# A GELU layer's output product: one float32 matmul each in place of three of rounded parts

## The chip, the cores and the metric

The kernel runs on one core of a Trainium2 chip. The metric is the device time of one execution in microseconds (us); lower is better. A core has TensorE (PE, whose weight loads are listed apart as PEld), VectorE (DVE), ScalarE (ACT), GpSimd (POOL) and SyncE (SP, which issues the DMAs). Matmuls write PSUM, which has eight banks of 128 partitions x 512 float32.

## The reference

A decayed attention (4 batches, 8 heads, 768 steps, head size 48) feeds a soft mixture of experts, and that feeds the layer that the change is in:

```python
def _moe2_ref(x, w_in, w_out):            # x: 3072 x 384, w_in: 384 x 2048, w_out: 2048 x 384
    h = x @ w_in
    g = h * (1.0 / (1.0 + np.exp(-1.702 * h)))
    return (g @ w_out).astype(np.float32)
```

All inputs and the output are float32.

## The kernel before, in words

The program is written out by hand, one instruction stream for each engine, with semaphores between them: `wait_ge(s, n)` blocks the engine until semaphore `s` has reached `n`, `.then_inc(s, 1)` raises it when the instruction is done. No scheduler moves anything. There are three stages: the attention, the mixture of experts, and the layer above, which is the last. Ahead of the last stage the kernel has folded `w_in` with the experts' output into `mst` (128 x 2048) and holds the combine weights of all tokens in `cst` (128 x 3072), so that h of 128 hidden channels and 512 tokens is one matmul.

The last stage goes through 3072 tokens in 6 blocks of TB = 512, and in each block through FF = 2048 hidden channels in FC = 16 chunks of 128. A step is one chunk of one block, so there are 96 steps; T = 32 of them (two blocks) are one pass of `two_blocks`, and three passes (ITS = 3) make the stage. In step s:

- PE computes h of step s+2 into bank 6 or 7 by one matmul (`hidden`).
- ACT turns it into g by the GELU activation, into one of NG = 4 slots of `gact` (`gelu`), which lies in the tile `ring`.
- DVE splits g of step s (`split`): `g_hi` is g rounded to float32r, `g_lo` is g minus `g_hi`, rounded likewise. Both are float32r, a 32-bit type with fewer mantissa bits for TensorE.
- PE adds w_out^T g to the output, 128 output channels (CM = 3 groups `o`) by 512 tokens in each of three banks: for each group wo_hi·g_hi, wo_lo·g_hi and wo_hi·g_lo, so 9 matmuls of 128 x 128 by 128 x 512.

`w_out` lies raw in `wraw` (two slots of `ring`, loaded by four DMAs on SP's queue, one semaphore `ld_wout` for each quarter). In the first block ACT rounds one chunk of it per step to `wo_hi` (`round_wout`) and DVE subtracts it to `wo_lo` (`low_wout`). PE's banks 0 to 2 and 3 to 5 take turns by block. After a block ACT copies the three banks to `ostage` (`evacuate`) and SP stores them. At the very end the last step runs group by group, so that ACT and DVE can copy each finished bank (`last_done`).

float32r matmuls also stand in `hidden` and in the two products with `spread`. All the other matmuls of the kernel, apart from the bfloat16 ones of `stay_warm`, take plain float32 operands; `t.transpose` is a matmul with the identity.

Of the kernel before, what the change touches and what calls it, by code (L numbers as in the profile page):

```python
# [16 lines left out]
def decay_attention_soft_moe_gelu_kernel(nc, rk_in, w0_in, nat_in, u_in, phi_in, w1_in, w2_in, win_in, wout_in, out_t):  # L17
# [17 lines left out]
    CM = phi_in.shape[1]  # L35
    DM = CM * P
# [6 lines left out]
    FC = FF // P  # L43
    NT = B * NC
    N = NT * P
    TB = 512
    T = 2 * FC
    ITS = N // (2 * TB)
# [7 lines left out]
    with top:  # L56
        def sb(stack, name, shape, dt=F32):
            return stack.enter_context(nc.sbuf_tensor(name, shape, dt))

        def sem(name):  # L60
            return top.enter_context(nc.semaphore(name))
# [73 lines left out]


        gen3 = ExitStack()
        wo_hi = sb(gen3, "wo_hi", [P, FC, DM], F32R)
        wo_lo = sb(gen3, "wo_lo", [P, FC, DM], F32R)
        NG = 4  # L140
        gact = ring[:, 1, 0:NG * TB].rearrange("p (a t) -> p a t", a=NG)
        g_split = sb(gen3, "g_split", [P, NG, 2, TB], F32R)
        g_hi, g_lo = (g_split[:, :, q, :] for q in range(2))
        ostage = ring[:, 0, 0:2 * CM * TB].rearrange("p (a o t) -> p a o t", a=2, o=CM)
        gen3.close()
        gen2.close()
# [1 line left out]
        wraw = ring[:, 6:8, :].rearrange("p a m -> p (a m)")  # L148

        bank = [top.enter_context(nc.psum_tensor(f"bank{i}", [P, BANK], F32)) for i in range(8)]  # L150
# [49 lines left out]
        FQ = FC // WQ  # L200
        ld_win = [sem(f"ld_win{m}") for m in range(CM)]
        ld_wout = [sem(f"ld_wout{q}") for q in range(WQ)]
# [47 lines left out]
        spread_set = sem("spread_set")  # L250
        spread_done = sem("spread_done")
        m_out = [sem(f"m_out{i}") for i in range(2)]
        wohi_done = sem("wohi_done")
        wolo_done = sem("wolo_done")

        h_done = sem("h_done")
        g_done = sem("g_done")
        ghi_done = sem("ghi_done")
        glo_done = sem("glo_done")
        step_done = sem("step_done")  # L260
        o_out = [sem(f"o_out{i}") for i in range(2)]
        last_done = sem("last_done")
# [195 lines left out]
        def _(act):  # L458
            a = nc.scalar
# [143 lines left out]
                combine_out(q, act, lambda dst, src: a.activation(dst, src, ACT.Copy), ct_act)  # L603

            a.preload_act_table(ACT.Gelu_apprx_sigmoid)
            def round_wout(f):
                if f % FQ == 0:
                    act.wait_ge(ld_wout[f // FQ], 16)
                a.activation(wo_hi[:, f, :], wraw[:, DM * f:DM * (f + 1)], ACT.Copy).then_inc(wohi_done, 1)

            act.wait_ge(l2_done, 1)
            combine(0)
            combine(1)
            act.wait_ge(m_done, 1)
            a.activation(mhi[:, :], bank[0][:, :], ACT.Copy).then_inc(m_hi, 1)
            combine(2)
            round_wout(0)
            for q in range(0, WQ, 2):
                act.wait_ge(spread_done, q + 1)
                a.activation(mst[:, q * BANK:(q + 1) * BANK], bank[SPREAD[q]][:, :], ACT.Copy).then_inc(m_out[0], 1)  # L620

            def gelu(it, s):
                act.wait_ge(h_done, T * it + s + 1)
                act.wait_ge(glo_done, T * it + s + 1)
                a.activation(gact[:, s % NG, :], bank[6 + s % 2][:, :], ACT.Gelu_apprx_sigmoid).then_inc(g_done, 1)  # L625

            def evacuate(it, par):
                act.wait_ge(step_done, T * it + FC * (par + 1) + NG)
                act.wait_ge(stored[par], 16 * it + 16)
                for o in range(CM):  # L630
                    a.activation(ostage[:, par, o, :], bank[3 * par + o][:, :], ACT.Copy).then_inc(o_out[par], 1)

            def two_blocks(it, last=False, rounding=False):
                for s in range(T):
                    if s + 2 < T or not last:
                        gelu(it, s + 2)
                    if rounding and s + 2 < FC:
                        round_wout(s + 2)
                    if rounding and s < 2:
                        combine(4 + s)  # L640
                    if s == FC:
                        evacuate(it, 0)
                if not last:
                    evacuate(it, 1)

            gelu(0, 0)
            gelu(0, 1)
            round_wout(1)
            two_blocks(0, rounding=True)
            with act.Fori(1, ITS - 1) as it:  # L650
                two_blocks(it)
            two_blocks(ITS - 1, last=True)
# [6 lines left out]
        @block.vector  # L659
        def _(dve):  # L660
            v = nc.vector
            dve.sem_inc(glo_done, NG)
            dve.sem_inc(logit_out, 1)
            v.memset(lw[:, :, D:HOFF], 0.0).then_inc(const_dve, 1)
            for q in (5, 6, 7):
# [178 lines left out]
            v.tensor_copy(si4[:, :], bank[6][:, 0:DM]).then_inc(so_out, 1)  # L844
            dve.wait_ge(so_t, 1)
            v.tensor_copy(soT[:, :, :], bank[7][:, 0:CM * NS].rearrange("p (m s) -> p m s", m=CM)).then_inc(so_ready, 1)
            def low_wout(f):
                dve.wait_ge(wohi_done, f + 1)
                v.tensor_tensor(wo_lo[:, f, :], wraw[:, DM * f:DM * (f + 1)], wo_hi[:, f, :].bitcast(F32),
                                ALU.subtract).then_inc(wolo_done, 1)  # L850

            dve.wait_ge(m_hi, 1)
            v.tensor_tensor(mlo[:, :], bank[0][:, :], mhi[:, :].bitcast(F32), ALU.subtract).then_inc(m_lo, 1)
            combine_out(3, dve, v.tensor_copy, ct_dve)
            low_wout(0)
            for q in range(1, WQ, 2):
                dve.wait_ge(spread_done, q + 1)
                v.tensor_copy(mst[:, q * BANK:(q + 1) * BANK], bank[SPREAD[q]][:, :]).then_inc(m_out[1], 1)

            def split(it, s):  # L860
                dve.wait_ge(g_done, T * it + s + 3)
                dve.wait_ge(step_done, T * it + s + 1)
                v.tensor_copy(g_hi[:, s % NG, :], gact[:, s % NG, :]).then_inc(ghi_done, 1)  # L863
                dve.wait_ge(ghi_done, T * it + s + 1)
                v.tensor_tensor(g_lo[:, s % NG, :], gact[:, s % NG, :], g_hi[:, s % NG, :].bitcast(F32), ALU.subtract).then_inc(glo_done, 1)  # L865

            for s in range(T):
                split(0, s)
                if s + 1 < FC:
                    low_wout(s + 1)  # L870
            with dve.Fori(1, ITS) as it:
                for s in range(T):
                    split(it, s)

            dve.wait_ge(last_done, 2)
            dve.wait_ge(stored[1], 16 * ITS)
# [2 lines left out]
        @block.tensor  # L879
        def _(pe):  # L880
            t = nc.tensor
            pe.sem_inc(step_done, NG)
            pe.sem_inc(lgt_done, 1)
            pe.sem_inc(logit_done, 1)

# [176 lines left out]
            last = Step(B - 1, PPB - 2)  # L1062
# [18 lines left out]
            for n in range(OLD):  # L1081
# [5 lines left out]
                if n == 3 * G4:  # L1087
                    pe.wait_ge(new_exp, 1)
                    for j in range(2):
                        ins = t.transpose(bank[2][:, G3 * NS * j:G3 * NS * (j + 1)], e_new[0:G3 * NS, P * j:P * (j + 1)],  # L1090
                                          ident[0:G3 * NS, 0:G3 * NS])
# [3 lines left out]
                ins = dispatch(bank[6], n, n < G4, n >= OLD - G4)  # L1095
            ins.then_inc(old_slots, 1)
            pe.wait_ge(new_weights, 1)
            for n in range(OLD, NT):
                ins = dispatch(bank[7], n, n < OLD + G4, n >= NT - G4)
# [6 lines left out]
            for m in range(CM):  # L1106
                ins = t.matmul(bank[0][:, NS * m:NS * (m + 1)], si4[:, P * m:P * (m + 1)], sel[:, 0:NS], start=True, stop=True)
# [94 lines left out]
            def two_blocks(it, last=False):  # L1202
                for s in range(T):
                    par, f = divmod(s, FC)
                    if s + 2 < T or not last:
                        hidden(it, s + 2)
                    if s == 0:
                        for i in range(2):
                            pe.wait_ge(m_out[i], WQ // 2)
                        pe.wait_ge(ct_dve, 1)  # L1210
                    if s == 4:
                        pe.wait_ge(ct_act, 5)
                    if f == 0:
                        pe.wait_ge(o_out[par], CM * it + 1)
                    pe.wait_ge(ghi_done, T * it + s + 1)
                    if last and s == T - 1:
                        pe.wait_ge(glo_done, T * it + s + 1 + NG)
                        for o in range(CM):
                            for wo, g in ((wo_hi, g_hi), (wo_lo, g_hi), (wo_hi, g_lo)):
                                ins = t.matmul(bank[3 * par + o][:, :], wo[:, f, P * o:P * (o + 1)], g[:, s % NG, :],  # L1220
                                               start=False, stop=(g is g_lo))
                            ins.then_inc(last_done, 1)
                        continue
                    for wo in (wo_hi, wo_lo):
                        if s < FC:
                            pe.wait_ge(wohi_done if wo is wo_hi else wolo_done, s + 1)
                        for o in range(CM):
                            t.matmul(bank[3 * par + o][:, :], wo[:, f, P * o:P * (o + 1)], g_hi[:, s % NG, :],  # L1228
                                     start=(f == 0 and wo is wo_hi), stop=False)
                    pe.wait_ge(glo_done, T * it + s + 1 + NG)  # L1230
                    for o in range(CM):
                        ins = t.matmul(bank[3 * par + o][:, :], wo_hi[:, f, P * o:P * (o + 1)], g_lo[:, s % NG, :],  # L1232
                                       start=False, stop=(f == FC - 1))
                    ins.then_inc(step_done, 1)

            hidden(0, 0)
            hidden(0, 1)
# [48 lines left out]
```

## Time and profile before

| | before |
|---|---|
| runs (us) | 406.31, 401.21, 403.70 |
| median of 3 | 403.7 |
| the profiled execution's own time | 402.38 |
| its span, first to last instruction | 400.7 |
| PE busy in the span | 392.0 us, 98% |
| mean granted TensorE clock | 1.000 |

The profiled execution's time is its span and 1.7 us around it. Times in the profile count from the start of the span. PE being busy 98% is modelled from overlapping matmuls: the mean ns of a matmul is its latency from start to end, and a new one starts before the last has ended, so the pace is read from starts, or from the length of a run of matmuls.

### The profile page before, as it was taken

What the parts mean: (1) busy time and instruction counts of PE and PEld (TensorE: products, weight loads), DVE (VectorE), ACT (ScalarE), POOL (GpSimd) and SP (SyncE); (2) the same over time, 40 slices, a digit from 0 to 9 for tenths busy, and PEclk for the clock granted to TensorE, in tenths of its full rate; (3) what the DMA queues carried; (4) which work ended last, traced back from release to release, by engine and by line L of the source; (5) the groups of instructions that cost most, each with busy time, mean ns of one, the idle gap of its engine ahead of it and who ended that gap; (6) DMA issues with size and microseconds to landing.
All of it is one profiled execution on the core that took longest, in us unless ns stands there. A gap on an engine that the chain in (4) does not pass through costs nothing.

```text
span 400.7 us, 8754 instructions
## 1 busy us (share of the span) xinstructions
PE 392.0 (98%) x3306; PEld 313.1 (78%) x3306; DVE 242.5 (61%) x453; ACT 188.7 (47%) x418; POOL 49.1 (12%) x50
## 2 busy tenths in 40 slices
PE   7998999999999999999999999999999999999996
PEld 6877888888888743458888888888888888888885
DVE  5877886977978766148675445454454545445451
ACT  5777877787788523055444222422332242223221
POOL 3522442224322200000000000000000000000000
PEclk9999999999999999999999999999999999999999
DMA  7999999899999899950000200200020020002002
GB/s 293 413 360 393 334 371 344 298 398 353 327 358 346 345 408 400 416 213 2 1 2 2 77 2 0 79 0 1 0 79 0 0 79 2 0 2 79 0 2 79
DMA packets 15859, 68.66 MB, mean 171 GB/s; under 512 B 1744, under 2 KB 2896, under 8 KB 14800
## 3 DMA queue, kind: packets, MB, share of 16 engines
q1 hardware_dynamic: 15824, 68.18, 44.5%
q8 instruction: 24, 0.39, 0.4%
q14 instruction: 11, 0.09, 0.1%
HBM read 63.46 MB, written 4.72 MB: 170 GB/s over the span
## 4 chain that ended last, share of the span: by engine, by line
PE 86%; DMA 7%; DVE 3%; issue 1%; ACT 1%; SPq 1%; DVEq 0%; ACTq 0%
PE bank L1228 32%; PE bank L1232 16%; PE bank L1199 6%; DMA rk<-rk_in 5%; PE bank L1008 4%; PE bank L894 4%; PE bank L1035 4%; PE bank L1128 3%; PE bank L1148 3%; PE bank L1027 2%; DMA nat<-nat_in 2%; PE bank L990 2%; PE bank L974 2%; PE bank L953 2%; PE bank L914 2%
## 5 line engine op out<-in xcount | busy, mean ns | idle before, releaser
L625 ACT ACTIVATE ring<-bank 128x512 f32<-128x512 f32 x96 | 57.4, 598 | 138.4 <-PE bank L1199 138.3
L863 DVE CAST g_split<-ring 128x512 fp32r<-128x512 f32 x96 | 40.8, 425 | 88.4 <-ACT ring L625 88.4
L1228 PE MATMUL bank<-g_split,wo_hi 128*128 128x512 f32 x285 | 80.1, 389 | 0.0
L1228 PE MATMUL bank<-g_split,wo_lo 128*128 128x512 f32 x285 | 80.0, 389 | 0.0
L1232 PE MATMUL bank<-g_split,wo_hi 128*128 128x512 f32 x285 | 80.0, 389 | 0.0
L865 DVE TENSOR_TENSOR g_split<-ring,g_split 128x512 fp32r<-128x512 f32 x96 | 66.5, 693 | 3.3
L1228 PEld LDWEIGHTS bank<-g_split,wo_hi 128*128 128x128 f32 x285 | 53.4, 188 | 11.2 <-DVE g_split L863 0.2
L1232 PEld LDWEIGHTS bank<-g_split,wo_hi 128*128 128x128 f32 x285 | 53.5, 188 | 11.1
L1228 PEld LDWEIGHTS bank<-g_split,wo_lo 128*128 128x128 f32 x285 | 53.5, 188 | 11.1
L1199 PE MATMUL bank<-cst,mst 128*128 (+1 forms) x96 | 37.4, 391 | 0.0
L443 POOL TENSOR_TENSOR nat<-nat 128x576 f32<-128x576 f32 x16 | 22.6, 1414 | 78.9 <-DVE nat L735 45.9
L715 DVE TENSOR_TENSOR at<-bank,causal 128x512 f32<-128x512 f32 x48 | 30.0, 680 | 1.5 <-PE bank L1008 1.5
L520 ACT ACTIVATE sc<-tsum,fdec 112x48 f32<-112x48 f32 x80 | 23.6, 372 | 9.9 <-DVE tsum L709 9.9
L1008 PE MATMUL bank<-rk 48*128 48x128 f32 x384 | 25.7, 280 | 0.0
L894 PE MATMUL bank<-tri,lw 128*112 128x129 f32 x192 | 25.2, 280 | 0.3 <-ACT lw L470 0.3
L1035 PE MATMUL bank<-at,nat 128*48 128x128 f32 x384 | 24.3, 276 | 0.0
L894 PEld LDWEIGHTS bank<-tri,lw 128*112 128x112 f32 x192 | 21.9, 177 | 2.4 <-ACT lw L470 0.6
L1008 PEld LDWEIGHTS bank<-rk 48*128 48x128 f32 x384 | 22.7, 187 | 1.2 <-issue 0.4
L698 DVE TENSOR_TENSOR rk<-rk,pinv 112x768 f32<-112x768 f32 x15 | 14.5, 966 | 14.7 <-DMA rk<-rk_in 9.8
L447 POOL TENSOR_TENSOR nat<-nat,ub 128x576 f32<-128x576 f32 x16 | 22.6, 1411 | 3.1 <-DVE tsum L709 2.0
L1035 PEld LDWEIGHTS bank<-at,nat 128*48 128x48 f32 x384 | 20.2, 123 | 3.0 <-issue 3.0
L1199 PEld LDWEIGHTS bank<-cst,mst 128*128 128x128 f32 x96 | 17.9, 188 | 3.9 <-ACT mst L620 0.3
(162 smaller groups left out, 429.7 us busy)
## 6 DMA issues: line engine op xcount, KB each, us to landing
nat<-nat_in SPq DMA_DIRECT2D x32, 576.0 KB, 5.8
rk<-rk_in SPq DMA_DIRECT2D x16, 768.0 KB, 7.5
ring<-w_in SPq DMA_DIRECT2D x16, 768.0 KB, 7.4
w2a<-w_in SPq DMA_DIRECT2D x4, 1536.0 KB, 8.9
out_t<-ring SPq DMA_DIRECT2D x5, 768.0 KB, 3.5
ring<-w_in SPq DMA_DIRECT2D x6, 512.0 KB, 7.2
ring<-win_in SPq DMA_DIRECT2D x3, 1024.0 KB, 7.9
ring<-wout_in SPq DMA_DIRECT2D x4, 768.0 KB, 13.6
```

The costliest lines, as they stand in the source:

```text
L443: g.tensor_tensor(rb, rb, kb, ALU.mult).then_inc(bonus_done, 1)
L520: ins = a.activation(sc[0:DP, c, :], tsum[0:DP, :].rearrange("p (e c) -> p e c", e=D)[:, :, c], ACT.Copy, scale=fdec[0:DP, c:c + 1])
L625: a.activation(gact[:, s % NG, :], bank[6 + s % 2][:, :], ACT.Gelu_apprx_sigmoid).then_inc(g_done, 1)
L715: v.tensor_tensor(at[:, 4 * q:4 * q + 4, :], bank[2 + q][:, :].rearrange("p (u t) -> p u t", u=4), causal[:, :].unsqueeze(1).to_broadcast( ...
L863: v.tensor_copy(g_hi[:, s % NG, :], gact[:, s % NG, :]).then_inc(ghi_done, 1)
L865: v.tensor_tensor(g_lo[:, s % NG, :], gact[:, s % NG, :], g_hi[:, s % NG, :].bitcast(F32), ALU.subtract).then_inc(glo_done, 1)
L894: return t.matmul(bank[c // G3][0:DP, (c % G3) * (P + 1):(c % G3 + 1) * (P + 1)], lw[:, c, 0:DP], tri[:, :], start=True, stop=True)
L1008: ins = t.matmul(bank[2 + u // 4][:, P * (u % 4):P * (u % 4 + 1)], k[rows, P * c:P * (c + 1)], r[rows, P * c:P * (c + 1)], start=True, sto ...
L1035: ins = t.matmul(bank[6 + q][half:half + D, P * (c // 2):P * (c // 2 + 1)], nat[s.slot][:, 0, HD * c + D * h:HD * c + D * (h + 1)], at[:, ...
L1199: t.matmul(bank[6 + s % 2][:, :], mst[:, P * f:P * (f + 1)], cst[:, bass.ds((2 * it + n) * TB, TB)], start=True, stop=True).then_inc(h_don ...
L1228: t.matmul(bank[3 * par + o][:, :], wo[:, f, P * o:P * (o + 1)], g_hi[:, s % NG, :], start=(f == 0 and wo is wo_hi), stop=False)
L1232: ins = t.matmul(bank[3 * par + o][:, :], wo_hi[:, f, P * o:P * (o + 1)], g_lo[:, s % NG, :], start=False, stop=(f == FC - 1))
```

## The change

It drops the tiles `wo_hi`, `wo_lo` and `g_split` and everything that fills them (`round_wout` on ACT, `low_wout` and `split` on DVE). PE multiplies `wraw` with `gact` directly, both plain float32, with one matmul for each group `o`. PE now waits for `gelu` itself (`g_done`) and, in the first block, for the quarter of w_out (`ld_wout`).

```diff
-            def split(it, s):
-                dve.wait_ge(g_done, T * it + s + 3)
-                dve.wait_ge(step_done, T * it + s + 1)
-                v.tensor_copy(g_hi[:, s % NG, :], gact[:, s % NG, :]).then_inc(ghi_done, 1)
-                dve.wait_ge(ghi_done, T * it + s + 1)
-                v.tensor_tensor(g_lo[:, s % NG, :], gact[:, s % NG, :], g_hi[:, s % NG, :].bitcast(F32), ALU.subtract).then_inc(glo_done, 1)
...
             def gelu(it, s):
                 act.wait_ge(h_done, T * it + s + 1)
-                act.wait_ge(glo_done, T * it + s + 1)
...
-                    pe.wait_ge(ghi_done, T * it + s + 1)
...
-                    for wo in (wo_hi, wo_lo):
-                        if s < FC:
-                            pe.wait_ge(wohi_done if wo is wo_hi else wolo_done, s + 1)
-                        for o in range(CM):
-                            t.matmul(bank[3 * par + o][:, :], wo[:, f, P * o:P * (o + 1)], g_hi[:, s % NG, :],
-                                     start=(f == 0 and wo is wo_hi), stop=False)
-                    pe.wait_ge(glo_done, T * it + s + 1 + NG)
-                    for o in range(CM):
-                        ins = t.matmul(bank[3 * par + o][:, :], wo_hi[:, f, P * o:P * (o + 1)], g_lo[:, s % NG, :],
-                                       start=False, stop=(f == FC - 1))
-                    ins.then_inc(step_done, 1)
+                    if s < FC and f % FQ == 0:
+                        pe.wait_ge(ld_wout[f // FQ], 16)
+                    pe.wait_ge(g_done, T * it + s + 3)
+                    for o in range(CM):
+                        ins = t.matmul(bank[3 * par + o][:, :], wraw[:, DM * f + P * o:DM * f + P * (o + 1)], gact[:, s % NG, :],
+                                       start=(f == 0), stop=(f == FC - 1))
+                        if last and s == T - 1:
                             ins.then_inc(last_done, 1)
+                    if not (last and s == T - 1):
+                        ins.then_inc(step_done, 1)
```

On PE, one step of the last stage stood like this before; `cst,mst` is `hidden`, the three rows of three are the products of rounded parts, and the ISA and REGISTER_ALU rows set up waits.

```order
L1199 MATMUL bank<-cst,mst 128x512
L1214 ISA
L1215 REGISTER_ALU
L1228 MATMUL bank<-g_split,wo_hi 128x512 x3
L1228 MATMUL bank<-g_split,wo_lo 128x512 x3
L1230 REGISTER_ALU
L1232 MATMUL bank<-g_split,wo_hi 128x512 x3
```

The same step in the changed program, to the next `hidden`; both operands of the product now lie in `ring`, and a row counts matmuls as they are written in the program:

```order
L1158 MATMUL bank<-cst,mst 128x512
L1173 ISA
L1178 MATMUL bank<-ring 128x512 x3
L1156 REGISTER_ALU
L1158 MATMUL bank<-cst,mst 128x512
```

The nine matmuls after `hidden` have become three. On DVE, the end of the folding and the first step of the last stage stood like this before:

```order
L853 TENSOR_TENSOR mlo<-bank,mhi 128x512
L307 CAST cst<-bank 128x512
L849 TENSOR_TENSOR wo_lo<-ring,wo_hi 128x384
L858 CAST mst<-bank 128x512 x2
L863 CAST g_split<-ring 128x512
L865 TENSOR_TENSOR g_split<-ring,g_split 128x512
```

And in the changed program, to the end of DVE's stream:

```order
L829 TENSOR_TENSOR mlo<-bank,mhi 128x512
L299 CAST cst<-bank 128x512
L833 CAST mst<-bank 128x512 x2
L837 COPY ring<-bank 128x512
L56 UNCONDITIONAL_BRANCH
```

The subtraction for `wo_lo` that stood ahead of the two copies to `mst` is gone, and after these copies DVE has only the last bank's copy left.

## Rows read from the trace of the kernel before

**Rows 1.** The page: busy time and instructions of each engine; granted clock in 40 slices

```profile
PE 392.0 (98%) x3306; PEld 313.1 (78%) x3306; DVE 242.5 (61%) x453; ACT 188.7 (47%) x418; POOL 49.1 (12%) x50
...
PEclk9999999999999999999999999999999999999999
```

**Rows 2.** The page: shares of the span in the chain that ended last

```profile
PE 86%; DMA 7%; DVE 3%; issue 1%; ACT 1%; SPq 1%; DVEq 0%; ACTq 0%
```

**Rows 3.** Stage table (x: instructions; then clock, DMA share, GB/s): last stage, its 80 steady steps

```profile
180.20:397.40 217.20, 217.17 (x958) 179.58 (x957) 114.19 (x207) 71.15 (x127) 0.00 (x0) 1.00 0.05 19
182.33:362.40 180.07, 180.07 (x796) 149.16 (x795) 95.76 (x175) 59.58 (x107) 0.00 (x0) 1.00 0.05 18
```

**Rows 4.** Timeline of PE: an early step, the next `hidden`, and one 80 steps on

```profile
182.33 0.39 PE L1199 MATMUL bank<-cst,mst 128*128 x1
182.56 0.84 PE L1228 MATMUL bank<-g_split,wo_hi 128*128 128x512 f32 x3
183.24 0.84 PE L1228 MATMUL bank<-g_split,wo_lo 128*128 128x512 f32 x3
183.92 0.84 PE L1232 MATMUL bank<-g_split,wo_hi 128*128 128x512 f32 x3
184.60 0.39 PE L1199 MATMUL bank<-cst,mst 128*128 x1
...
363.67 0.39 PE L1199 MATMUL bank<-cst,mst 128*128 128x512 f32 x1
```

**Rows 5.** Matmul groups by shape (stationary partitions*columns, moving): count, busy, latency

```profile
L1228 PE MATMUL bank<-g_split,wo_hi 128*128 128x512 f32 x285 | 80.1, 389 | 0.0
L1128 PE MATMUL bank<-ring,slotT 128*32 128x512 f32 x96 | 10.7, 594 | 0.1
L1174 PE MATMUL bank<-ring,soT 128*32 128x512 f32 x24 | 2.8, 596 | 0.0
L1148 PE MATMUL bank<-w2a,hidT 128*32 128x384 f32 x64 | 5.8, 489 | 0.0
L894 PE MATMUL bank<-tri,lw 128*112 128x129 f32 x192 | 25.2, 280 | 0.3 <-ACT lw L470 0.3
L1156 PE MATMUL bank<-ident,cs 128*128 128x128 f32 x24 | 3.6, 281 | 0.0
```

**Rows 6.** Timeline of PE: uninterrupted runs of float32 matmuls, start and length

```profile
147.59 7.07 PE L1128 MATMUL bank<-ring,slotT 128*32 128x512 f32 x64
...
159.07 2.76 PE L1148 MATMUL bank<-w2a,hidT 128*32 128x384 f32 x32
...
172.91 2.78 PE L1174 MATMUL bank<-ring,soT 128*32 128x512 f32 x24
...
67.08 1.57 PE L894 MATMUL bank<-tri,lw 128*112 128x129 f32 x12
```

**Rows 7.** Weight loads by tile: duration ns min/median/max, first and last start, forms

```profile
L894 PEld LDWEIGHTS bank<-tri,lw x192: 172/177/177, 4.4 to 124.8; 128*112 128x112 f32 x192
L1008 PEld LDWEIGHTS bank<-rk x384: 182/188/188, 9.2 to 132.6; 48*128 48x128 f32 x192
L1228 PEld LDWEIGHTS bank<-g_split,wo_hi x285: 186/188/189, 180.2 to 393.4; 128*128 128x128 f32 x143
L891 PEld LDWEIGHTS bank<-ones x33: 95/99/181, 1.3 to 178.1; 128*128 128x128 bf16 x33
```

**Rows 8.** Groups of DVE and ACT in the last stage; idle before, and its releaser

```profile
L865 DVE TENSOR_TENSOR g_split<-ring,g_split 128x512 fp32r<-128x512 f32 x96 | 66.5, 693 | 3.3
L863 DVE CAST g_split<-ring 128x512 fp32r<-128x512 f32 x96 | 40.8, 425 | 88.4 <-ACT ring L625 88.4
L849 DVE TENSOR_TENSOR wo_lo<-ring,wo_hi 128x384 fp32r<-128x384 f32 x16 | 8.9, 557 | 7.7 <-ACT wo_hi L609 7.7
L625 ACT ACTIVATE ring<-bank 128x512 f32<-128x512 f32 x96 | 57.4, 598 | 138.4 <-PE bank L1199 138.3
L609 ACT ACTIVATE wo_hi<-ring 128x384 fp32r<-128x384 f32 x16 | 8.3, 519 | 0.0
L631 ACT ACTIVATE ring<-bank 128x512 f32<-128x512 f32 x15 | 7.9, 601 | 2.9 <-PE bank L1232 2.9
```

**Rows 9.** The chain in order of time into the last stage: start, us, what

```profile
178.48 0.73 PE bank L1199 x2
179.21 0.87 PE bank L1156 x8
180.08 0.24 PE bank L1199
180.32 1.49 PE bank L1228 x6
```

**Rows 10.** Issues and landings of the four DMAs that load w_out

```profile
L388 SPq DMA_DIRECT2D ring<-wout_in x4: 422/432/543, 160.2 to 161.7; - x4
...
DMA to landing us min/median/max: 11.5/13.6/15.6
```

More of the change, by code:

```diff
@@ L137, in decay_attention_soft_moe_gelu_kernel @@
         gen3 = ExitStack()
-        wo_hi = sb(gen3, "wo_hi", [P, FC, DM], F32R)
-        wo_lo = sb(gen3, "wo_lo", [P, FC, DM], F32R)
         NG = 4
         gact = ring[:, 1, 0:NG * TB].rearrange("p (a t) -> p a t", a=NG)
-        g_split = sb(gen3, "g_split", [P, NG, 2, TB], F32R)
-        g_hi, g_lo = (g_split[:, :, q, :] for q in range(2))
         ostage = ring[:, 0, 0:2 * CM * TB].rearrange("p (a o t) -> p a o t", a=2, o=CM)
@@ L252, in decay_attention_soft_moe_gelu_kernel @@
         m_out = [sem(f"m_out{i}") for i in range(2)]
-        wohi_done = sem("wohi_done")
-        wolo_done = sem("wolo_done")
         h_done = sem("h_done")
         g_done = sem("g_done")
-        ghi_done = sem("ghi_done")
-        glo_done = sem("glo_done")
         step_done = sem("step_done")
@@ L605, in _ @@
             a.preload_act_table(ACT.Gelu_apprx_sigmoid)
[L606 to L609, printed above, removed]
             act.wait_ge(l2_done, 1)
@@ L616, in _ @@
             combine(2)
-            round_wout(0)
             for q in range(0, WQ, 2):
@@ L623, in gelu @@
                 act.wait_ge(h_done, T * it + s + 1)
-                act.wait_ge(glo_done, T * it + s + 1)
                 a.activation(gact[:, s % NG, :], bank[6 + s % 2][:, :], ACT.Gelu_apprx_sigmoid).then_inc(g_done, 1)
             def evacuate(it, par):
-                act.wait_ge(step_done, T * it + FC * (par + 1) + NG)
+                act.wait_ge(step_done, T * it + FC * (par + 1))
                 act.wait_ge(stored[par], 16 * it + 16)
@@ L631, in evacuate, with two_blocks @@
                     a.activation(ostage[:, par, o, :], bank[3 * par + o][:, :], ACT.Copy).then_inc(o_out[par], 1)
-            def two_blocks(it, last=False, rounding=False):
+            def two_blocks(it, first=False, last=False):
                 for s in range(T):
@@ L636, in two_blocks @@
                         gelu(it, s + 2)
-                    if rounding and s + 2 < FC:
-                        round_wout(s + 2)
-                    if rounding and s < 2:
+                    if first and s < 2:
                         combine(4 + s)
@@ L647, in _ @@
             gelu(0, 1)
-            round_wout(1)
-            two_blocks(0, rounding=True)
+            two_blocks(0, first=True)
             with act.Fori(1, ITS - 1) as it:
@@ L661, in _ @@
             v = nc.vector
-            dve.sem_inc(glo_done, NG)
             dve.sem_inc(logit_out, 1)
@@ L846, in _ @@
             v.tensor_copy(soT[:, :, :], bank[7][:, 0:CM * NS].rearrange("p (m s) -> p m s", m=CM)).then_inc(so_ready, 1)
[L847 to L850, printed above, removed]
             dve.wait_ge(m_hi, 1)
@@ L854, in _ @@
             combine_out(3, dve, v.tensor_copy, ct_dve)
-            low_wout(0)
             for q in range(1, WQ, 2):
@@ L858, in _ @@
                 v.tensor_copy(mst[:, q * BANK:(q + 1) * BANK], bank[SPREAD[q]][:, :]).then_inc(m_out[1], 1)
-            def split(it, s):
-                dve.wait_ge(g_done, T * it + s + 3)
-                dve.wait_ge(step_done, T * it + s + 1)
-                v.tensor_copy(g_hi[:, s % NG, :], gact[:, s % NG, :]).then_inc(ghi_done, 1)
-                dve.wait_ge(ghi_done, T * it + s + 1)
-                v.tensor_tensor(g_lo[:, s % NG, :], gact[:, s % NG, :], g_hi[:, s % NG, :].bitcast(F32), ALU.subtract).then_inc(glo_done, 1)
[L867 to L873, printed above, removed]
             dve.wait_ge(last_done, 2)
@@ L881, in _ @@
             t = nc.tensor
-            pe.sem_inc(step_done, NG)
             pe.sem_inc(lgt_done, 1)
@@ L1214, in two_blocks @@
                         pe.wait_ge(o_out[par], CM * it + 1)
-                    pe.wait_ge(ghi_done, T * it + s + 1)
-                    if last and s == T - 1:
-                        pe.wait_ge(glo_done, T * it + s + 1 + NG)
-                        for o in range(CM):
-                            for wo, g in ((wo_hi, g_hi), (wo_lo, g_hi), (wo_hi, g_lo)):
-                                ins = t.matmul(bank[3 * par + o][:, :], wo[:, f, P * o:P * (o + 1)], g[:, s % NG, :],
-                                               start=False, stop=(g is g_lo))
-                            ins.then_inc(last_done, 1)
-                        continue
-                    for wo in (wo_hi, wo_lo):
-                        if s < FC:
-                            pe.wait_ge(wohi_done if wo is wo_hi else wolo_done, s + 1)
-                        for o in range(CM):
-                            t.matmul(bank[3 * par + o][:, :], wo[:, f, P * o:P * (o + 1)], g_hi[:, s % NG, :],
-                                     start=(f == 0 and wo is wo_hi), stop=False)
-                    pe.wait_ge(glo_done, T * it + s + 1 + NG)
-                    for o in range(CM):
-                        ins = t.matmul(bank[3 * par + o][:, :], wo_hi[:, f, P * o:P * (o + 1)], g_lo[:, s % NG, :],
-                                       start=False, stop=(f == FC - 1))
-                    ins.then_inc(step_done, 1)
+                    if s < FC and f % FQ == 0:
[5 more added lines that the diff above has]
+                        if last and s == T - 1:
+                            ins.then_inc(last_done, 1)
+                    if not (last and s == T - 1):
+                        ins.then_inc(step_done, 1)
             hidden(0, 0)
```

## The prediction

> **What bounds the kernel now.** I read the page first: PE is busy 98% of the span at the full granted clock [rows 1], and the chain that ended last lies 86% on PE [rows 2]. That share alone doesn't say what the last stage is worth, so I went on to the stage table: from 180.20 to 397.40, PE is busy 217.17 of 217.20 us, at clock 1.00, with DVE at 114 us and ACT at 71 us [rows 3]. More than half of the execution is this stage, and in it nothing but PE's own pace counts. The pace is read from the starts, since the listed 389 ns is a latency [rows 5]: `hidden` starts at 182.33 and, 80 steps later, at 363.67 [rows 4]. That is 2.267 us for a step of ten float32r matmuls, **0.2267 us for each**, and one early step is as long (184.60 − 182.33 = 2.27). The reader is to see that no step waits for the split, for rounding or for a store, so work taken from DVE and ACT gives nothing back.
>
> **What the change removes from DVE and ACT.** 96 pairs of cast and subtraction (40.8 + 66.5 us), 16 subtractions (8.9 us) and 16 roundings on ACT (8.3 us) go [rows 8]. All of it lies beside a PE that is never idle, so its worth on the path is 0. ACT keeps 96 GELUs of 0.598 us [rows 8] and waits 138 us in all for `hidden`; it stays far from being late. PE's new wait is for `gelu` of step s, but `hidden(s+2)`, which stands ahead of it in PE's queue, already waited for the same count. Nothing new is queued behind it, and this costs 0. PE's wait for a quarter of w_out costs 0 as well: the last of the four loads is issued at 161.7 and the longest takes 15.6 us to land [rows 10], so all are there by 177.3, before the first product near 180.3 [rows 9].
>
> **What it does to PE.** 96 × 9 float32r matmuls go and 96 × 3 float32 ones come; `hidden` (96, float32r) stays. The question is the price of a float32 product of 128 x 128 by 512. No row has that shape with the array's full width, so I take it apart.
>
> First, how many instructions one product is. The program has 6 matmuls at L894 for each of 16 pairs, 96 in all, and the trace lists 192; at L1174 it has 12 and the trace lists 24; at L1128, 48 and 96 [rows 5]. float32 products run as two instructions. float32r products don't: 285 of a possible 288 at L1228 are listed for wo_hi [rows 5], and the stage has 958 instructions on PE for ten a step [rows 3]. Transposes don't either (24 written, 24 listed at L1156), but they aren't products.
>
> Second, the pace of one such instruction. At L1128 four matmuls of 32 output columns run side by side, so 64 instructions are 16 turns of the moving 512 columns: (7.07 − 0.594) / 15 = 0.4317 us a turn. At L1174, 6 turns of the same: (2.78 − 0.596) / 5 = 0.4368. With 384 columns at L1148, 8 turns: (2.76 − 0.489) / 7 = 0.3244 [rows 5, 6]. From 384 to 512 columns the cost grows by 0.00084 us a column, about twice what a float32r column can cost (0.2267 / 512 = 0.00044). For the full width the nearest row is L894 with 112 output columns and 129 moving: (1.57 − 0.280) / 11 = 0.1173 [rows 5, 6], where the line through L1128 and L1148 gives 0.3244 − 255 × 0.00084 = 0.1107 (an estimate). The wide weights thus add some 0.0066. So the ends for a turn at full width are 0.432 (nothing added) and 0.443 (L1174 with 0.0066 added), and I take **0.437**, L1128 with most of that added.
>
> The sum for a step: 3 products × 2 × 0.437 = 2.622 against 9 × 0.2267 = 2.040, that is +0.582 us; for 96 steps **+55.9 us**. By the ends of the turn it is 96 × (2.592 − 2.040) = +53.0 and 96 × (2.658 − 2.040) = +59.3.
>
> The Trainium skill (TensorE: Matmul & The Clock Gate, Back-to-back issue gap) gives the start-to-start of a warm matmul as N / 2.4 + 2.5 ns. For N = 512 that is 216 ns, 11 ns less than this trace's 227 for float32r. An estimate by that page for a product of four passes is 4 × 213.3 + 2 × 2.5 = 858 ns, for which the sum would be 96 × (3 × 0.858 − 2.040) = +51 us instead of +56. The measured pace decides, and so the sum goes by the rows above.
>
> **Both ends of the stage.** At the opening DVE's 0.557 us subtraction ahead of the copies to `mst` goes, and so does the first cast. But the chain shows PE working without a gap through the transposes and `hidden` into the first product [rows 9], so at most some 0.4 us comes back, and I take 0. At the end the last product's latency is 594 instead of 389 ns [rows 5], +0.2 us. Copies and store follow as before. ACT's three copies after a block and a GELU take 3 × 0.601 + 0.598 = 2.4 us [rows 8], longer than a step of 2.27 and shorter than one of 2.85; there was no gap on PE before, and there will be none.
>
> The sum against the profiled execution's own 402.38 us: 402.38 + 55.9 + 0.2 = **458.5 us**. The median of the runs shown is 403.7, so the profiled one is 0.3% quicker than that; the runs lie between 401.2 and 406.3.
>
> **Rivals.**
>
> *A product costs less than three float32r matmuls (faster).* The mechanism is that a wide float32 product runs as one instruction of 0.437, as the transposes do (24 of 24 at L1156). A step is then 3 × 0.437 + 0.227 = 1.54 us, 70 us less in all: 332 us. Should the operands be taken as float32r after all, so that the change doesn't do what it says, it is 4 × 0.2267 = 0.907 a step, 131 us less: 272 us. The case turns to faster from the point at which a product costs under 3 × 0.2267 = 0.680, so 0.340 an instruction if there are two. For it speaks only that no row has the full shape. Against it: every float32 line that isn't a transpose is listed twice, L894 with 112 columns among them, and all turns of 512 take 0.432 or more [rows 5, 6]. Chance 4%.
>
> *Weight loads come into the open (slower still).* A float32 product loads two sets of weights. A load takes 0.188 us [rows 7] and is hidden now, since a float32r matmul and its load together take 0.2267. If the second half's load couldn't run under the first half's matmul, 288 × 0.188 = 54 us come on top: 512 us; if none could, 108 us: 566 us. Against it: at L894 a float32 instruction comes every 0.117 us although its load alone takes 0.177, and a longer matmul gives more cover, not less. Chance 4%. The Trainium skill (the same page, Part 3, The mechanism) states that a weight load overlaps a running matmul only if it is for another row group, which would be this rival in full, and would hold for float32r too; the trace speaks against it. It also says (Weight-path perf modes) that the fast weight load is on when the type isn't FP32. The bfloat16 load takes 99 ns here and float32r's 188, as float32's [rows 7], so the change loses no fast load.
>
> *The clock falls to its lower level, 1.2 GHz.* It was at 2.4 GHz (1.00) in every slice [rows 1, 3], in float32 stages as in float32r ones, with PE always at work. If the whole stage ran at half clock, 96 × 2.85 = 273 us would be added: about 731 us. Chance 1%.
>
> **How the numbers follow.** The forecast has 90%: 458.5 us, slower. The ends of the turn and of the opening give 402.38 + 53.0 − 0.4 = 455 and 402.38 + 59.3 + 0.2 = 462; the runs of before reach 0.3% below the profiled one and 1.0% above, which makes 453.6 to 466.5. The skill's price lies a little under that, and I let the range go from 451 to 467. The faster rival has 4%, exposed loads 4%, the clock 1%, and 1% is for something that cancels most of it. That makes faster by over 2% 0.04, within 2% (about what a measurement can tell from no change here) 0.01, slower 0.95.
>
> **What the profile after would show.** The product's line has twice its 288 matmuls, near 576, with a latency near 594 ns. `hidden` starts every 2.85 us. PE stays without idle time until the end, the stage is about 273 us long, DVE is idle in it but for one copy, and ACT's wait for `hidden` grows by some 55 us. Everything ahead of 180 us stays as it is. I am wrong if that line has 288 entries, if steps are under 2.27 us, if PE idles between products for ACT or for its own weight loads, or if the granted clock leaves 1.00.

## The result, and the profile after

| | before | changed |
|---|---|---|
| median (us) | 403.32 (4 runs, 401.21 to 406.31) | 454.31 (4 runs, 454.09 to 455.22) |
| the profiled execution | 402.38, span 400.7 | 455.22, span 453.5 |

The ratio is **1.126** (95% interval 1.119 to 1.134): the change makes the kernel 51 us slower. The forecast was 458.5 us in a range of 451 to 467.

The first lines are the changed kernel's page: busy time and instructions of each engine, the granted clock in 40 slices, the chain's shares, and the groups of the product and of the GELU.

```profile
PE 444.9 (98%) x3018; PEld 261.0 (58%) x3018; DVE 127.9 (28%) x245; ACT 182.4 (40%) x402; POOL 49.0 (11%) x50
...
PEclk9999999999999999999999999999999999999999
...
PE 89%; DMA 6%; DVE 3%; issue 1%; SPq 1%; ACT 1%; DVEq 0%; POOL 0%; POOLq 0%
PE bank L1178 55%; DMA rk<-rk_in 6%; PE bank L1158 5%; PE bank L967 4%; PE bank L853 4%; PE bank L994 3%; PE bank L1087 2%; PE bank L1107 2%; PE bank L986 2%; PE bank L933 2%; PE bank L949 2%; PE bank L912 1%; PE bank L892 1%; PE bank L873 1%; PE bank L850 1%; PE bank L1019 1%
...
L1178 PE MATMUL bank<-ring 128*128 128x512 f32 x576 | 262.5, 592 | 0.0
...
L610 ACT ACTIVATE ring<-bank 128x512 f32<-128x512 f32 x96 | 57.2, 597 | 193.6 <-PE bank L1158 193.5
```

Against [rows 1]: DVE's busy time has halved, 98% of the span is still PE, and the new line alone holds 55% of the chain. The 288 products are 576 instructions. ACT waits 193.5 us for `hidden` where it waited 138.3 [rows 8]: what was taken from the other engines has become their idle time.

The next lines are the changed kernel's timeline of PE: two steps, and the end, where 18 instructions of the product run without a `hidden` between them.

```profile
183.56 0.80 PE L1158 MATMUL bank<-cst,mst 128*128 x1
184.20 2.74 PE L1178 MATMUL bank<-ring 128*128 128x512 f32 x6
186.37 0.79 PE L1158 MATMUL bank<-cst,mst 128*128 x1
...
441.78 0.79 PE L1158 MATMUL bank<-cst,mst 128*128 128x512 f32 x1
442.41 7.89 PE L1178 MATMUL bank<-ring 128*128 128x512 f32 x18
```

From 183.56 to 441.78 are 92 steps: **2.807 us a step** against 2.267 in [rows 4]. That is +0.540, and 96 × 0.540 = +51.8 us, the whole of the loss. The last line gives the pace of one instruction undisturbed: (7.89 − 0.592) / 17 = **0.4293 us**, so 0.859 us a product where three float32r matmuls took 0.680. What is left for `hidden` is 2.807 − 6 × 0.4293 = 0.231, a little over its 0.2267 among its own kind.

The weight loads of the changed kernel, in the timeline with what each load engine waited for, don't come into the open:

```profile
300.14 0.19 PEld L1178 LDWEIGHTS bank<-ring 128*128 128x128 f32 x1 [0.24 <-issue]
300.57 0.19 PEld L1178 LDWEIGHTS bank<-ring 128*128 128x128 f32 x1 [0.24 <-issue]
```

Each lasts 0.19 us and starts 0.43 us after the last, with 0.24 us of idle time between, while the matmuls show no gap (0.0 us idle at L1178 in the page above): there is one load for each of a product's two instructions, and it runs under the instruction before it.

### The profile page after: what moved, and what is told of

Same layout as the page of the kernel before. It is cut to its first block, busy times and chain, and to the rows that moved or that the text cites. A ratio compares the mean times of both kernels' runs of the same rounds, so it can differ in the third digit from the quotient of the medians.

```text
span 453.5 us, 7646 instructions
## 1 busy us (share of the span) xinstructions
PE 444.9 (98%) x3018; PEld 261.0 (58%) x3018; DVE 127.9 (28%) x245; ACT 182.4 (40%) x402; POOL 49.0 (11%) x50
## 4 chain that ended last, share of the span: by engine, by line
PE 89%; DMA 6%; DVE 3%; issue 1%; SPq 1%; ACT 1%; DVEq 0%; POOL 0%; POOLq 0%
PE bank L1178 55%; DMA rk<-rk_in 6%; PE bank L1158 5%; PE bank L967 4%; PE bank L853 4%; PE bank L994 3%; PE bank L1087 2%; PE bank L1107 2%; PE bank L986 2%; PE bank L933 2%; PE bank L949 2%; PE bank L912 1%; PE bank L892 1%; PE bank L873 1%; PE bank L850 1%; PE bank L1019 1%
## 5 line engine op out<-in xcount | busy, mean ns | idle before, releaser
L1178 PE MATMUL bank<-ring 128*128 128x512 f32 x576 | 262.5, 592 | 0.0
L1178 PEld LDWEIGHTS bank<-ring 128*128 128x128 f32 x576 | 109.3, 190 | 119.0 <-issue 115.0
L610 ACT ACTIVATE ring<-bank 128x512 f32<-128x512 f32 x96 | 57.2, 597 | 193.6 <-PE bank L1158 193.5
L1158 PE MATMUL bank<-cst,mst 128*128 (+1 forms) x96 | 75.2, 785 | 0.0
L679 DVE TENSOR_TENSOR rk<-rk,pinv 112x768 f32<-112x768 f32 x15 | 14.4, 960 | 15.2 <-DMA rk<-rk_in 10.2
L556 ACT ACTIVATE yts<-bank 112x384 f32<-112x384 f32 x32 | 15.7, 491 | 3.6 <-PE bank L994 2.5
L487 ACT ACTIVATE pinv<-bank 112x387 f32<-112x387 f32 x30 | 13.1, 490 | 8.3 <-PE bank L853 8.1
L933 PE MATMUL bank<-ident,rk 112*128 112x112 f32 x96 | 12.2, 262 | 2.8 <-DVE rk L679 2.3
L681 DVE TENSOR_TENSOR rk<-rk,pw 112x768 f32<-112x768 f32 x15 | 14.3, 951 | 0.0
L986 PE MATMUL bank<-rk,sc 48*48 48x128 f32 x320 | 13.8, 277 | 0.2
```

What stands on the lines that cost most here:

```text
L933: ins = t.transpose(bank[bk][:, DP * col:DP * (col + 1)], k[0:DP, P * c:P * (c + 1)], ident[0:DP, 0:DP])
L986: ins = t.matmul(bank[6 + c % 2][half:half + D, P * (c // 2):P * (c // 2 + 1)], sc[rows, c - 1, :], r[rows, P * c:P * (c + 1)], start=(c < ...
L1158: t.matmul(bank[6 + s % 2][:, :], mst[:, P * f:P * (f + 1)], cst[:, bass.ds((2 * it + n) * TB, TB)], start=True, stop=True).then_inc(h_don ...
L1178: ins = t.matmul(bank[3 * par + o][:, :], wraw[:, DM * f + P * o:DM * f + P * (o + 1)], gact[:, s % NG, :], start=(f == 0), stop=(f == FC ...
```

## The experiments

Times stand against the kernel before as run with each set: 403.6 us for the first four, 403.4 for the next four, 403.05 for the last three.

### The split work is kept, and nobody reads it

DVE's `split` and `low_wout` and ACT's `round_wout` of the kernel before stay; only PE's product is the changed one.

```diff
-                    pe.wait_ge(ghi_done, T * it + s + 1)
+                    pe.wait_ge(g_done, T * it + s + 3)
...
+                        ins = t.matmul(bank[3 * par + o][:, :], wraw[:, DM * f + P * o:DM * f + P * (o + 1)], gact[:, s % NG, :],
+                                       start=(f == 0), stop=(f == FC - 1))
```

> PE multiplies float32 by float32 as in the changed kernel, but ACT still rounds w_out and DVE still splits g, and nobody reads the results. Theory (only PE's own pace counts): 454 us, as without that work, step 2.81 us. Rival (the work of DVE and ACT slows PE's reads, which would explain why a float32r matmul takes 0.2267 us for 512 columns): a float32 instruction streams for twice as long, so up to 576 x 0.022 = 12 us more, 466 us.

454.53 us (ratio 1.125, 1.119 to 1.131). Its PE timeline:

```profile
331.64 0.79 PE L1199 MATMUL bank<-cst,mst 128*128 x1
332.27 2.74 PE L1219 MATMUL bank<-ring 128*128 128x512 f32 x6
334.45 0.80 PE L1199 MATMUL bank<-cst,mst 128*128 x1
```

A step is 2.81 us with DVE at work and without. So the removal of all rounding and splitting is worth nothing that can be measured (454.31 against 454.53 us), and the whole loss belongs to PE's matmuls.

### Only one of three output groups in float32

```diff
+                    whole(par, f, s)
...
-                        for o in range(CM):
+                        for o in range(1, CM):
```

`whole` is the changed kernel's matmul of `wraw` and `gact` for group 0; both loops over the rounded parts begin with group 1.

> Only output group 0 is multiplied in float32 (one matmul a step); groups 1 and 2 keep the three float32r matmuls. Theory (prices add): a product costs 2 x 0.4293 = 0.859 in place of 0.680 us, so 96 x 0.179 = 17 us over before, about 420.5 us, step 2.446. Rival (changing between the types costs time on its own): more than 2% above that, over 429 us.

425.45 us (1.054, 1.047 to 1.061), so 5 us over the sum and between the two forecasts. The timeline of PE:

```profile
329.69 0.40 PE L1199 MATMUL bank<-cst,mst 128*128 x1
329.93 1.02 PE L1203 MATMUL bank<-ring 128*128 128x512 f32 x2
330.38 1.04 PE L1235 MATMUL bank<-g_split,wo_hi 128*128 128x512 f32 x2
331.26 0.62 PE L1235 MATMUL bank<-g_split,wo_lo 128*128 128x512 f32 x2
331.72 0.63 PE L1239 MATMUL bank<-g_split,wo_hi 128*128 128x512 f32 x2
332.18 0.39 PE L1199 MATMUL bank<-cst,mst 128*128 x1
```

A step is 332.18 − 329.69 = 2.49 (2.480 as the mean of 60 steps). If the float32 product takes its 0.859, 1.62 is left for seven float32r matmuls: 0.232 each on average, and not 0.2267. That is 96 × 7 × 0.005 = 3.4 of the missing 5 us; the rest was not located. The size is otherwise as expected: a third of the products gives 22 us.

### The parts as bfloat16

```diff
-        wo_hi = sb(gen3, "wo_hi", [P, FC, DM], F32R)
-        wo_lo = sb(gen3, "wo_lo", [P, FC, DM], F32R)
+        wo_hi = sb(gen3, "wo_hi", [P, FC, DM], BF16)
+        wo_lo = sb(gen3, "wo_lo", [P, FC, DM], BF16)
...
-        g_split = sb(gen3, "g_split", [P, NG, 2, TB], F32R)
+        g_split = sb(gen3, "g_split", [P, NG, 2, TB], BF16)
```

> The kernel before with the rounded parts of g and of w_out as bfloat16 in place of float32r; still three matmuls a product. Theory (the 0.013 us that a float32r matmul takes over its 0.213 us of streaming is the price of a 0.188 us weight load behind it, and bfloat16 loads take 0.099): a matmul near 0.216 us, 864 x 0.011 = 9.5 us less than before, about 394 us. Rival (the surplus comes from the stream itself or from DVE's traffic): 0.2267 still, 403 us.

**395.79 us** (0.979, 0.973 to 0.985), faster than both kernels: the interval leaves no doubt that it is faster, but not whether by 2%. A product still takes three matmuls, but of parts with fewer bits. The timeline of PE:

```profile
331.40 0.58 PE L1199 MATMUL bank<-cst,mst 128*128 128x512 f32 x1
331.82 0.82 PE L1228 MATMUL bank<-g_split,wo_hi 128*128 128x512 bf16 x3
...
333.13 0.81 PE L1232 MATMUL bank<-g_split,wo_hi 128*128 128x512 bf16 x3
333.59 0.58 PE L1199 MATMUL bank<-cst,mst 128*128 128x512 f32 x1
```

(0.81 − 0.379) / 2 = 0.2155 us a matmul, as expected (0.379 is the latency of one); the step is 2.187 as a mean of the stage. Of the 9 × 0.011 = 0.10 saved a step, `hidden`, still float32r but now among bfloat16 matmuls, takes back 0.02 (2.187 − 9 × 0.2158 = 0.245). The time was right; the reason given for it (the length of the weight load) is tested by `halves` and `narrow` below, and falls.

### Float32 products in halves and in quarters

```diff
-                        ins = t.matmul(bank[3 * par + o][:, :], wraw[:, DM * f + P * o:DM * f + P * (o + 1)], gact[:, s % NG, :],
+                        for half in (slice(0, TB // 2), slice(TB // 2, TB)):
...
+                            ins = t.matmul(bank[3 * par + o][:, half], wraw[:, DM * f + P * o:DM * f + P * (o + 1)], gact[:, s % NG, half],
```

`quarters` has four slices of TB // 4 in place of the two.

> The changed kernel with each float32 product in two matmuls of 256 columns, so 12 instructions a step of 0.213 us of streaming in place of 6 of 0.427. Theory (the surplus hangs on a 0.188 us load beside 0.213 us of streaming, whatever the type): 0.2267 each as for float32r, step 12 x 0.2267 + 0.227 = 2.947, 96 x 0.14 = 13.5 us over the changed kernel, 468 us. Rival (a fixed 0.0025 us for each instruction): 455.7 us.

456.22 us (1.134, 1.126 to 1.142): the rival. The timeline:

```profile
331.82 0.59 PE L1158 MATMUL bank<-cst,mst 128*128 x1
332.25 2.75 PE L1180 MATMUL bank<-ring 128*128 128x256 f32 x12
334.65 0.59 PE L1158 MATMUL bank<-cst,mst 128*128 x1
```

(2.75 − 0.379) / 11 = 0.2155 us an instruction, half of 0.4293 and 0.001 more. A load of 0.190 us for every instruction of 0.2155 us costs float32 nothing. So the load's length alone doesn't make a float32r matmul take 0.2267.

> The changed kernel with each float32 product in four matmuls of 128 columns, 24 instructions a step. In halves an instruction took 0.2166 us, 0.0033 over its streaming. If the 0.1173 us that the wide rows with 129 columns showed is a matter of short streams: 24 x 0.1165 + 0.23 = 3.03 a step, about +21 us on the changed kernel, 475 us. If each instruction adds 0.0033 whatever its length: 24 x 0.110 + 0.23 = 2.87, about +6 us, 460 us.

472.71 us (1.172, 1.167 to 1.177), near the first figure but not for its reason. The timeline at the turn from the first pass of the loop to the second:

```profile
271.61 0.48 PE L1158 MATMUL bank<-cst,mst 128*128 x1
271.93 2.84 PE L1180 MATMUL bank<-ring 128*128 128x128 f32 x24
276.55 0.49 PE L1158 MATMUL bank<-cst,mst 128*128 x1 [1.78 <-issue]
276.88 1.11 PE L1180 MATMUL bank<-ring 128*128 128x128 f32 x5
279.52 4.42 PE L1180 MATMUL bank<-ring 128*128 128x128 f32 x19 [1.53 <-issue]
283.60 0.68 PE L1158 MATMUL bank<-cst,mst 128*128 x1
```

(2.84 − 0.276) / 23 = 0.1115 us an instruction. A step away from the turn is 2.913 us, so 96 × 0.106 = 10 us over the changed kernel. At the turn PE stands still twice, for 1.78 and 1.53 us, waiting for nothing that the profile shows. Behind the first of these gaps the granted clock falls to 0.50, the level of 1.2 GHz, from some 277 to 284 us; 19 instructions take 4.42 us there, where 24 take 2.84. Gaps and clock together make the three steps from 271.61 on 6.4 us too long. The profiled execution took 472.04 us, 16.8 over the changed kernel's 455.22, and 10.2 + 6.4 account for it. The window with the low clock (the clock stands before the DMA share and GB/s) and the instruction queue of this run's page:

```profile
278.00:284.00 6.00, 4.48 (x20) 4.48 (x21) 0.00 (x0) 0.00 (x0) 0.00 (x0) 0.50 0.28 105
...
q8 instruction: 40, 0.66, 0.6%
```

The instruction queue moves 0.66 MB, where the changed kernel moves 0.36. A longer loop body that has to be fetched again would explain the gaps; that is not shown, since no run here varies the body alone.

### Does DVE's traffic or the load's width set the float32r pace?

`no_split` has float32r matmuls and an idle DVE: the GELU writes g rounded, and a product multiplies the same two rounded tiles three times, leaving out the low parts; it is made from the changed kernel, and its diff stands first. `narrow` is the kernel before with 96 instead of 128 stationary columns, leaving out 32 of each 128 output channels.

```diff
+        gact = sb(gen3, "gact", [P, NG, TB], F32R)
...
+                        for n in range(3):
+                            ins = t.matmul(bank[3 * par + o][:, :], wo_hi[:, f, P * o:P * (o + 1)], gact[:, s % NG, :],
```

```diff
-                            t.matmul(bank[3 * par + o][:, :], wo[:, f, P * o:P * (o + 1)], g_hi[:, s % NG, :],
+                            t.matmul(bank[3 * par + o][0:96, :], wo[:, f, P * o:P * o + 96], g_hi[:, s % NG, :],
```

> Nine float32r matmuls a step as before, but all three of a product multiply the same rounded g (written by the GELU) with the same rounded w_out, so the low parts are left out and DVE does nothing in the stage. Theory (DVE's and ACT's traffic doesn't touch PE's pace): 0.2267 us each still, step 2.267, 403 us. Rival (a float32r matmul loses 0.011 us to DVE's traffic): 0.216 each, about 393.5 us.

404.1 us (1.002, 0.999 to 1.004), with steps of 2.27 us: DVE's traffic plays no part, and the pace is PE's own.

> The kernel before with stationary operands of 96 columns in place of 128 in the nine products, so 32 of each 128 output channels are left out; the streaming stays 512 columns. Theory (what a float32r matmul takes over 0.2158 hangs on its weight load's length): load 0.141 us in place of 0.188, a matmul between 0.216 and 0.224, 394 to 401 us. Rival (the surplus belongs to float32r's stream): 0.2267, 403 us.

407.73 us (1.011, 1.007 to 1.016), slower than either figure. Two groups of its table of shapes:

```profile
L1228 PE MATMUL bank<-g_split,wo_hi 128*96 128x512 f32 x234 | 67.5, 397 | 0.0
...
L1228 PEld LDWEIGHTS bank<-g_split,wo_hi 128*96 128x96 f32 x234 | 37.9, 162 | 15.2
```

And its timeline of PE:

```profile
332.88 0.40 PE L1199 MATMUL bank<-cst,mst 128*128 128x512 f32 x1
333.11 0.86 PE L1228 MATMUL bank<-g_split,wo_hi 128*96 128x512 f32 x3
333.81 0.85 PE L1228 MATMUL bank<-g_split,wo_lo 128*96 128x512 f32 x3
334.50 0.85 PE L1232 MATMUL bank<-g_split,wo_hi 128*96 128x512 f32 x3
335.20 0.40 PE L1199 MATMUL bank<-cst,mst 128*128 128x512 f32 x1
```

The load is shorter (0.162 for 0.188), but the step is longer, 2.32 us, 0.232 a matmul. The surplus isn't paid at the change of width alone: within the nine narrow matmuls each group of three takes 0.69 to 0.70 us. Together with `halves` this rejects the load's length as the cause. Why a float32r matmul takes 0.2267 us among full-width ones and 0.232 beside other shapes or types stays open.

### Column tiles

```diff
-                        ins = t.matmul(bank[3 * par + o][:, :], wraw[:, DM * f + P * o:DM * f + P * (o + 1)], gact[:, s % NG, :],
+                        for j in range(0, P, 32):
+                            ins = t.matmul(bank[3 * par + o][j:j + 32, :], wraw[:, DM * f + P * o + j:DM * f + P * o + j + 32],
...
```

> The changed kernel with each float32 product as four matmuls of 32 output columns side by side. This is the shape of the rows from which the lower end of the prediction came. If those rows are a fair price of their shape: 0.4317 to 0.4368 a turn against 0.4292 of the full width, so 1.4 to 4.4 us over the changed kernel, 455.7 to 458.7 us. If full width and column tiles cost the same: 454.3 us.

490.59 us (1.217, 1.212 to 1.221), far over both figures. Its timeline of PE:

```profile
330.58 0.50 PE L1158 MATMUL bank<-cst,mst 128*128 x1
331.01 2.78 PE L1179 MATMUL bank<-ring 128*32 128x512 f32 x24
333.72 0.49 PE L1158 MATMUL bank<-cst,mst 128*128 x1
```

The timeline of its weight loads, in the same step:

```profile
331.01 0.16 PEld L1179 LDWEIGHTS bank<-ring 128*32 128x32 f32 x8 [0.24 <-issue]
331.46 0.13 PEld L1179 LDWEIGHTS bank<-ring 128*32 128x32 f32 x4 [0.30 <-issue]
331.89 0.13 PEld L1179 LDWEIGHTS bank<-ring 128*32 128x32 f32 x4 [0.30 <-issue]
```

The loads of one turn follow those of the last by 0.43 us, just as with full width; only the first turn is 0.45. The step is 3.14: less 6 × 0.4293, `hidden` costs 0.56 instead of 0.23, and what is new around it is that the matmuls beside it are column tiles, so that the tiling changes twice a step. That is 96 × 0.33 = 32 of the 36 us. The stall at the loop's turn is here too, with two gaps of 1.0 and 1.5 us; in the profiled execution it costs some 5 us. And these rows show what was wrong with reading the pace from a run's length: (2.78 − 0.592) / 5 = 0.4376 is too high by 0.04 us spread over five turns: 0.02 is the late first turn, and the other 0.02 fits the last three matmuls of a turn ending after the first.

### `hidden` in float32 too, and fewer parts

```diff
-        cst = sb(gen2, "cst", [P, N], F32R)
+        cst = sb(gen2, "cst", [P, N])
...
-        mst = sb(gen2, "mst", [P, FF], F32R)
+        mst = sb(gen2, "mst", [P, FF])
```

`two_parts` and `one_part` are made from `no_split`: the first multiplies `gact` by `wo_hi` and by `wo_lo`, which DVE fills in the first block, the second by `wo_hi` alone.

```diff
-                        for n in range(3):
+                        for n, wo in enumerate((wo_hi, wo_lo)):
```

```diff
-                        for n in range(3):
+                        for n in range(1):
```

> The changed kernel with mst and cst in float32 too, so that hidden is a fourth float32 product a step and PE never changes the type within the stage. If a product costs 2 x 0.4292 = 0.858 us wherever it stands: step 8 x 0.4292 = 3.434, 96 x 0.627 = 60 us over the changed kernel, 514.5 us. If the step of 2.807 hides a price for changing the type twice a step, this comes out some us lower.

516.36 us (1.281, 1.274 to 1.287). The timeline:

```profile
300.13 1.02 PE L1158 MATMUL bank<-cst,mst 128*128 x2
...
303.56 1.02 PE L1158 MATMUL bank<-cst,mst 128*128 x2
```

3.43 us a step is 8 × 0.4293, and 516.36 lies 2 us over the sum. A product costs 0.859 wherever it stands, so the changed kernel's step hides no price for changing the type beyond the 0.004 us by which `hidden` there (0.231) lies over its 0.2267.

> Two float32r matmuls a product: w_out stays whole in two parts, g is rounded once by the GELU, so the product with g's low part is left out. If prices add: 7 x 0.2267 = 1.587 a step, 96 x 0.680 = 65 us under the kernel before, 338 us. If another engine gets in the way (in the first block ACT has a GELU of 0.598 and a rounding of 0.519 a step): a few us more.

338.45 us (0.839, 0.834 to 0.843), as the sum has it: six product matmuls a step instead of nine, and each one left out is worth its 0.2267.

> One float32r matmul a product, of rounded g and rounded w_out; both low parts are left out. This is the rival of the prediction in which the operands are taken as float32r after all. If prices add: 4 x 0.2267 = 0.907 a step, 131 us under the kernel before, 273 us. In the first block ACT needs 0.598 + 0.519 = 1.12 us a step, so PE should wait there, some 3 to 5 us in all: 276 to 278 us.

277.33 us (0.690, 0.684 to 0.696). Here another engine shows for the first time; PE's timeline while ACT evacuates a block:

```profile
243.10 0.84 PE L1190 MATMUL bank<-gact,wo_hi 128*128 128x512 f32 x3
244.28 0.50 PE L1169 MATMUL bank<-cst,mst 128*128 128x512 f32 x1 [0.34 <-ACT gact L618]
```

Steps are 0.907 us, and at a block's end `hidden` waits for the GELU that stands behind ACT's three copies: here 243.10 to 244.28 is 1.18 us, where 0.68 is usual. By the starts of `hidden`, the five turns between blocks cost 2.7 of the 4 us over 273, and the first block, where the wait was expected, 0.7. In that block a GELU and a rounding together start every 0.89 us by the timeline of ACT, though their durations add up to 1.25. They overlap, so the durations listed for single instructions don't add up to ACT's pace:

```profile
186.70 0.66 ACT L618 ACTIVATE gact<-bank 128x512 fp32r<-128x512 f32 x1
...
187.18 0.59 ACT L603 ACTIVATE wo_hi<-ring 128x384 fp32r<-128x384 f32 x1
...
187.59 0.66 ACT L618 ACTIVATE gact<-bank 128x512 fp32r<-128x512 f32 x1
```

`one_part` is the fastest version, but its output is of rounded operands alone. Of those that keep three products of parts, bfloat16 parts are the fastest.

## Why the prediction was right

**The bound.** That only PE's pace counts in the last stage was right, and is shown: with the split work kept the time is the same to 0.2 us (`keep_split`), and with the split left out at nine float32r matmuls too (`no_split`). PE's new waits cost nothing: the product's line shows 0.0 us of idle time ahead of it.

**The count.** Two instructions for a float32 product, read from the doubled lines [rows 5], became 576 at L1178. The faster rival would have needed 288.

**The term that was mis-sized** is the pace of a turn of 512 columns at full width: 0.437 taken, between 0.432 and 0.443, and 0.4293 measured, below the lower end. 576 × 0.0077 = 4.4 us; `hidden`'s slower 0.231 gives 0.4 back, and 55.9 − 4.4 + 0.4 = 51.9 is the 51.8 that the steps show. The result, 454.31, lies under the 455 to which the ends of the terms added up; it is inside the range because the spread of the runs (453.6) and the other estimate (451) widened it.

Both ends lay too high, for two reasons. The lower came from run lengths [rows 6], which in column tiles contain some 0.04 us that isn't pace (`col_tiles`); without it L1128's 16 turns give (7.07 − 0.594 − 0.04) / 15 = 0.4291. And the 0.0066 for the width doesn't exist at 512 columns, where full width and column tiles both take 0.43. Where L894's surplus comes from is only in part known: in `quarters` a full-width instruction of 128 columns takes 0.1115, where the line through 0.4293 and 0.2155 gives 0.2155 − 0.1069 = 0.1086, so 0.003 belongs to the short stream. L894's 0.117 for 129 columns is 0.005 over even that; what adds it wasn't tried.

The estimate from the Trainium skill's gap (TensorE: Matmul & The Clock Gate, Back-to-back issue gap), which the prediction set aside, came closer: 858 ns a product, and 859 was measured. The same gap fits bfloat16 (216 ns, and 215.5 here), and float32r lies 11 ns over it. But the section calls it the gap of an isolated matmul and gives some 131 ns for a sustained stream of 512 columns; no such stream here is faster than 215.5 ns a matmul.

**The rivals.** Weight loads stay covered, as the load rows after show, and in `halves` they stay covered at one load for every 0.2155 us. The Trainium skill's rule that a load overlaps only with matmuls of another row group (the same page, Part 3, The mechanism) doesn't hold in these traces, where loads and matmuls all take 128 rows; the text above the rule in that section also allows it for a background weight buffer, which fits. The clock stayed at 2.4 GHz in the changed kernel (1.00 in the stage). The price given for operands taken as float32r, 272 us, was tried as `one_part`: 277.

**The ends of the stage.** Nothing came back at the opening. Before, PE's first two `hidden` start at 178.48 [rows 9] and the stage's first product at 180.2 [rows 3]; after, by the timeline of PE, it is 179.70 and 181.38, as far apart:

```profile
179.70 0.73 PE L1158 MATMUL bank<-cst,mst 128*128 128x512 f32 x2
...
181.38 1.04 PE L1178 MATMUL bank<-ring 128*128 128x512 f32 x2
```

The 1.2 us by which all of it is later belong to the earlier stages, in this one execution. They are why its span grew by 52.8 us and the steps by only 51.8. What the profile was to show came: 576 entries of 592 ns, ACT's wait longer by 55 us, PE without idle time; the stage, 269 us from 181.38 to the last product's end, is shorter than the 273 forecast by the same mis-sized pace.

## What to carry to other kernels

On an engine that is never idle, multiply the count of its instructions by their pace, and take the pace from starts in a long uniform run, not from the length of a short one. At 128 x 128 x 512 a float32 product costs 0.859 us, three float32r matmuls 0.680, three bfloat16 ones 0.647; here rounding and splitting on engines with time to spare was free. Ask how many parts the result needs before asking how to multiply them: leaving out the first float32r part gave 66 us here (404.1 to 338.45), the second 61, mostly since ACT then began to hold PE up.

## What the runs showed of the hardware that was not expected

- Full-width and column-tiled float32 matmuls stream at the same pace (0.43 us for 512 columns), but a full-width float32r matmul between column tiles cost 0.33 us more than among full-width ones (`col_tiles`).
- A float32r matmul of 512 columns takes 0.2267 us where bfloat16 takes 0.2155, and so does one of the two instructions of a float32 product of 256 columns, with as long a weight load. With 96 instead of 128 stationary columns it takes 0.232, not less.
- With 24 float32 instructions a step (12 matmuls as written), PE stood still twice at the loop's turn, for 1.8 and 1.5 us in `quarters`, and the granted clock then stood at 0.50 for some 6 us. With 12 instructions a step (`halves`) there was no such gap.
- Two consecutive instructions of ACT overlap: a GELU of 0.66 us and a rounding of 0.59 us start together every 0.89 us (`one_part`).
